# A fused attention and MLP kernel: chunks of 320 and 256 tokens, one chunk apart, and a layer norm by a matmul of ones

## What is computed

```python
scores = where(0 <= i - j < 128, q @ k.T / 8 - slope[h] * abs(i - j), -1e9)   # i, j: tokens
attn = softmax(scores)                      # exp(s - max) / (sum + 1e-9)
x = (attn @ v), heads side by side          # 576 x 512 for each batch
xn = (x - mean(x)) / sqrt(var(x) + 1e-6) * g_ln
y = x + relu(xn @ w_ch1) @ w_ch2            # 512 -> 2048 -> 512
h = relu(y @ w_in)                          # 512 -> 1024
c = conv_w[0]*h[t-1] + conv_w[1]*h[t] + conv_w[2]*h[t+1]
out = (h * sigmoid(c)) @ w_out              # 1024 -> 512
```

## Time and profile before

| | us |
|---|---|
| median of 3 runs | 835.26 (834.32 to 838.26) |
| span of the profiled execution | 834.8 |
| prologue, to the first MLP matmul | 89.0 |
| MLP of batch 0, with attention of batch 1 | 151.5 |
| MLP of batch 1, with attention of batch 2 | 140.3 |
| MLP of batch 2, with attention of batch 3 | 138.6 |
| MLP of batch 3 | 104.1 |
| second network | 211.4 |

### The profile page before, as it was taken

One profiled execution on the slowest core, in us unless ns is written; L12 is line 12 of the kernel. 1 busy time (PEld: TensorE's weight loads), 2 busy tenths in 40 slices (PEclk: granted clock), 3 DMA queues, 4 the chain that ended last, 5 costly groups with the idle time before them and its releaser, 6 DMA issues.

```text
span 834.8 us, 17035 instructions
## 1 busy us (share of the span) xinstructions
PE 786.3 (94%) x5792; PEld 765.4 (92%) x5792; DVE 547.0 (66%) x1510; ACT 385.0 (46%) x1063; POOL 171.7 (21%) x155
## 2 busy tenths in 40 slices
PE   4776788999999999999999999999999999999998
PEld 3665778999999999998999999999998999999998
DVE  4997677777367777645677754522229887788862
ACT  5775456565224655512556632122235444444442
POOL 4553675211011211101112200021120110111100
PEclk9676799999999999999999999999999999999999
DMA  5441554221122123013121201411312122221101
GB/s 154 106 130 48 156 162 127 60 78 43 58 65 66 38 71 101 8 58 102 29 71 51 86 8 61 134 58 54 89 49 76 31 79 78 78 78 47 59 22 44
DMA packets 64425, 60.81 MB, mean 73 GB/s; under 512 B 23904, under 2 KB 52576, under 8 KB 63840
## 3 DMA queue, kind: packets, MB, share of 16 engines
q1 hardware_dynamic: 64352, 59.87, 24.3%
HBM read 45.69 MB, written 14.16 MB: 72 GB/s over the span
## 4 chain that ended last, share of the span: by engine, by line
PE 69%; DVE 11%; issue 11%; POOL 3%; ACT 2%; DMA 2%; SPq 1%; POOLq 0%; DVEq 0%; ACTq 0%
PE bank L1009 20%; PE bank L1011 19%; PE bank L1010 19%; PE bank L950 4%; PE bank L964 3%; PE bank L980 3%; DVE prob L741 2%; DVE q_st L829 1%; DMA w_stage<-w 1%; DMA q_raw<-qT 1%; DVE ch_stage L741 1%; POOL rstd L482 1%; DVE rows L734 1%; ACT prob L562 1%; DVE rows L736 1%
## 5 line engine op out<-in xcount | busy, mean ns | idle before, releaser
L1009 PE MATMUL bank<-h_hi,wb_hi 128*128 128x288 f32 x512 | 156.9, 306 | 3.1 <-DVE h_lo L798 2.3
L1009 PE MATMUL bank<-xn_hi,wa_hi 128*128 128x288 f32 x512 | 157.0, 307 | 2.7 <-issue 1.4
L1010 PE MATMUL bank<-xn_lo,wa_hi 128*128 128x288 f32 x512 | 152.0, 297 | 0.0
L1011 PE MATMUL bank<-xn_hi,wa_lo 128*128 128x288 f32 x512 | 152.0, 297 | 0.0
L1011 PE MATMUL bank<-h_hi,wb_lo 128*128 128x288 f32 x512 | 151.6, 296 | 0.0
L1010 PE MATMUL bank<-h_lo,wb_hi 128*128 128x288 f32 x512 | 151.5, 296 | 0.0
L798 DVE SCALAR_TENSOR_TENSOR h_lo<-bank,h_hi 128x288 fp32r<-128x288 f32 x128 | 58.1, 454 | 109.8 <-ACT h_hi L594 108.5
L594 ACT ACTIVATE h_hi<-bank 128x288 fp32r<-128x288 f32 x128 | 52.3, 409 | 164.1 <-PE bank L1011 163.1
L1009 PEld LDWEIGHTS bank<-h_hi,wb_hi 128*128 128x128 f32 x512 | 97.1, 190 | 5.2 <-issue 3.9
L1009 PEld LDWEIGHTS bank<-xn_hi,wa_hi 128*128 128x128 f32 x512 | 97.6, 191 | 4.0 <-issue 3.2
L1010 PEld LDWEIGHTS bank<-xn_lo,wa_hi 128*128 128x128 f32 x512 | 97.7, 191 | 0.0
(11 more groups left out here) (95 smaller groups left out, 1752.0 us busy)
## 6 DMA issues: line engine op xcount, KB each, us to landing
k_raw<-kT SPq DMA_DIRECT2D x64, 144.0 KB, 2.8
q_raw<-qT SPq DMA_DIRECT2D x64, 144.0 KB, 2.9
w_stage<-w SPq DMA_DIRECT2D x32, 256.0 KB, 3.0
x_in<-x_spill SPq DMA_DIRECT2D x8, 580.0 KB, 4.3
ch_in<-ch_spill SPq DMA_DIRECT2D x8, 580.0 KB, 5.2
x_spill<-xT SPq DMA_DIRECT2D x4, 1152.0 KB, 5.3
ch_spill<-ch_stage SPq DMA_DIRECT2D x32, 144.0 KB, 1.9
out<-out_stage SPq DMA_DIRECT2D x32, 144.0 KB, 1.8
```

The costliest lines, as they stand in the source:

```text
L1009: nc.tensor.matmul(dst, w_h, a_h, start=start, stop=False)
L1010: nc.tensor.matmul(dst, w_h, a_l, start=False, stop=False)
L1011: last = nc.tensor.matmul(dst, w_l, a_h, start=False, stop=stop)
```

## The change

**Chunks.** The tokens of a batch are now cut at 320 (T = 320, 256), for attention as for the MLP. Chunk 0 has the queries 0 to 319 with the keys 0 to 319 (three tiles), chunk 1 the queries 320 to 575 with the keys 192 to 575 (two tiles). Attention runs one chunk ahead of the MLP, not one batch. The prologue holds attention of batch 0's chunk 0; `first` the MLP of that chunk with attention of chunk 1; a loop of three turns has the phases `one` (MLP on 256 tokens of batch b, attention on 320 of batch b + 1) and `zero` (MLP on 320, attention on 256); `last` is the last MLP of 256 tokens. Heads are 3.2 slots apart in a phase of 32 slots, and a head's transposes stand 2.4 slots, its outputs 3.8 slots behind its scores. Raw q and k, v_st and prob have two buffers each; pt_hi, pt_lo and o_lo one.

**Layer norm.** GpSimd and VectorE sum xT over its four blocks of channels (x_sum); a float32 matmul with a matrix of 1/512 gives the mean in every partition; VectorE subtracts it (xc), and xc itself is split into xc_hi and xc_lo and goes into the MLP. ScalarE squares xc, GpSimd sums, a second such matmul gives the variance. It goes through three small DMAs and a power on 64 partitions to a row of 1/std for all partitions (move_var, store_rstd, load_rstd), which multiplies the MLP's output (it may, as relu commutes with a positive factor): two blocks on VectorE out of PSUM, two on GpSimd after a copy by ScalarE. GpSimd then adds xT, and the sum is stored once (y_spill), so that the second network loads one input and sums nothing.

**Weights.** 8 tiles are prepared in the prologue, 24 in `first`.

```diff
-LT = 96
-NORM_TIMES = {("IN", 0): 0.0, ("IN", 1): 1.0, ("OUT", 0): 3.0, ("IN", 2): 3.51, ("OUT", 1): 4.5, ("OUT", 2): 5.5}
-FIRST_NORM, FIRST_HEAD, HEAD_SLOTS, LAST_NORM = 0.0, 6.5, 5.2, 55.5
-LAG = {"S": 0, "PT": 1, "O": 1}
-W_PROLOGUE = 10
+T = (320, 256)
+TILES = ([(128, 0, 128, 128, 0), (128, 0, 256, 0, 128), (64, 128, 192, 0, 384)],
+         [(128, 0, 256, 0, 0), (128, 128, 256, 0, 256)])
+HEAD0, HEAD_SLOT = 0.8, 3.2
+AT = {("S", 0): 0.0, ("S", 1): 0.3, ("PT", 0): 2.4, ("O", 0): 3.8}
+VAR_AT, MEAN_AT = 6.0, 28.0
+AT_PROLOGUE = {("S", 0): 0.0, ("S", 1): 0.02, ("PT", 0): 1.04, ("O", 0): 1.4}
+W_PROLOGUE = 8
...
+        def phases(run, eng):
+            run("prologue", None, 0)
+            run("first", 0, 0)
+            with eng.Fori(0, B - 1) as b:
+                run("one", b, b + 1)
+                run("zero", b + 1, b + 1)
+            run("last", B - 1, None)
...
+            def mean(kind, bm, b):
...
+                nc.tensor.matmul(dst[:, 0:T[c]], ones[:], x_sum[:, 0:T[c]], start=True, stop=True).then_inc(bank_filled, 1)
+            def variance(kind, bm, ba):
...
+                nc.tensor.matmul(dst[:, 0:T[c]], ones[:], xc[:, 0, 0:T[c]], start=True, stop=True).then_inc(bank_filled, 1)
...
+            def sum_squares(b, c):
+                g = chunk_no(b, c)
+                pool.wait_ge(square_ready, g + 1)
+                nc.gpsimd.tensor_tensor(xc[:, 0:2, 0:T[c]], xc[:, 0:2, 0:T[c]], xc[:, 2:4, 0:T[c]], ALU.add).then_inc(square_step, 1)
+                pool.wait_ge(square_step, 2 * g + 1)
+                nc.gpsimd.tensor_tensor(xc[:, 0, 0:T[c]], xc[:, 0, 0:T[c]], xc[:, 1, 0:T[c]], ALU.add).then_inc(square_step, 1)
...
+            def add_residual(b, c):
...
+                pool.wait_ge(ch_act, g + 1)
+                pool.wait_ge(rstd_loaded, 16 * (g + 1))
+                nc.gpsimd.tensor_tensor(y_stage[:, 2:4, 0:T[c]], y_stage[:, 2:4, 0:T[c]],
+                                        rstd[:, 0:T[c]].unsqueeze(1).broadcast_to((P, 2, T[c])), ALU.mult).then_inc(ch_scaled, 1)
...
+                nc.gpsimd.tensor_tensor(y_stage[:, :, 0:T[c]], y_stage[:, :, 0:T[c]], xT[:, :, t0:t1], ALU.add).then_inc(y_done, 1)
...
+            def centre(b, c):
...
+                for part in range(2):
+                    nc.vector.tensor_tensor(xc[:, 2 * part:2 * part + 2, 0:T[c]], xT[:, 2 * part:2 * part + 2, T0[c]:T0[c] + T[c]],
+                                            src[:, 0:T[c]].unsqueeze(1).broadcast_to((P, 2, T[c])), ALU.subtract).then_inc(xc_ready, 1)
...
+            def evacuate(b, c):
...
+                nc.vector.tensor_tensor(y_stage[:, 0:2, 0:T[c]], acc[:, 0:2, 0:T[c]],
+                                        rstd[:, 0:T[c]].unsqueeze(1).broadcast_to((P, 2, T[c])), ALU.mult).then_inc(ch_dve, 1)
```

More of the change, by code:

```diff
@@ L98, in norm_items @@
[L98 to L115, removed]
@@ L144, in mlp_groups @@
 def mlp_groups():
[L146 to L149, removed]
+    seq = [("A", 0), ("A", 1)]
+    for k in range(2, F1):
+        seq += [("B", k - 2), ("A", k)]
+    seq += [("B", F1 - 2), ("B", F1 - 1)]
     return [(g - 1 + half / 2, x + (half,)) for g, x in enumerate(seq) for half in (0, 1)]
+MLP_C = {"first": 0, "one": 1, "zero": 0, "last": 1}
+ATT_C = {"prologue": 0, "first": 1, "one": 0, "zero": 1}
 def timeline(kind):
@@ new lines, with use_base @@
+USES = {k: [x for _, x in timeline(k) if x[0] in ("S", "PT", "O", "MEAN", "VAR")]
+        for k in ("prologue", "first", "one", "zero", "last")}
+assert USES["first"] == USES["zero"]
+N_USES = {k: len(v) for k, v in USES.items()}
+PAIR = N_USES["one"] + N_USES["zero"]
+assert N_USES["first"] % 2 == 0 and N_USES["one"] % 2 == 0
+def use_base(kind, batch):
+    if kind == "prologue":
+        return 0
+    first = N_USES["prologue"]
+    if kind == "first":
+        return first
+    first += N_USES["first"]
+    if kind in ("one", "last"):
+        return first + PAIR * batch
+    return first + PAIR * (batch - 1) + N_USES["one"]
@@ L415, in _ @@
+            phases(run, sp)
             last = B - 1
@@ L520, in run @@
                         y_lo_part(a[0], a[0])
-            run("prologue", 0)
-            run("first", 0)
-            with pool.Fori(0, B - 2) as b:
-                run("steady", b + 1)
-            run("last", B - 1)
+                    if kind == "first" and name == "v_lo" and a[0] == 0:
+                        sum_squares(0, 0)
+            phases(run, pool)
+            add_residual(B - 1, 1)
             with pool.Fori(0, B - 1) as b:
@@ new lines, in prob_t_hi, with phase_of @@
+            def prob_t_hi(b, c, h):
+                hd = head_no(b, c, h)
+                if (n := before(b, c, h, "O")) is not None:
+                    act.wait_ge(bank_filled, n)
+                act.wait_ge(bank_filled, last_use(b, c, ("PT", h, 0)))
+                src = bank[bank_no(phase_of(b, c), ("PT", h, 0))]
+                nc.scalar.activation(pt_hi[:], src[:], ACT.Copy).then_inc(pt_hi_ready, 1)
+            def phase_of(b, c):
+                if isinstance(b, int) and b == 0:
+                    return "first" if c else "prologue"
+                return "zero" if c else "one"
```

1072 lines of the change are left out of this document (539 added, 533 removed).

## The result

The changed kernel takes 919.85 us (median of 4 runs, 916.87 to 922.79) against 835.43 of the kernel before beside it: a ratio of 1.101 with the interval 1.097 to 1.104, slower by 10%. The profiled execution has a span of 914.7 us, 79.9 more than before. The direction was forecast and the size was not: 854 was the number, 875 the end of the range.

A forecast was written before the change was run, and what follows sets the result against it. TensorE was taken as busy throughout the last MLP and second network, the prologue as bound otherwise. 834.8 - 11 + 13 - 17.5 + 6.6 + 22.5 + 6 + 0 + 1.4 + 1 - 3 = 853.8, so 854 us; range 827 to 875.

The forecast's parts named there:

- The cadence of 320 and 256 columns: MLP on TensorE: matmuls of 320 columns come 0.146 us apart, those of 256 columns 0.12.
- MLP matmuls at zero: MLP: 384 matmuls each of 320 and 256 columns cost the same as 768 of 288, change zero.
- The attention of batch 0's second chunk, +13: Chunk 1 of batch 0 leaves the prologue and enters TensorE's stream: 8 heads x 14 x about 0.116, +13.0 us.
- the old transposes: Layer norm: groups of 4 transposes leave TensorE's stream, 2.5 us a chunk for 7 chunks, -17.5 us.
- the new matmuls: Layer norm: 15 products with the matrix of ones enter TensorE's stream at 0.44 us each, +6.6 us (2 to 13).
- The prologue: Prologue on 320 tokens becomes one chain of 8.1 us a head; MLP starts at 78 us (73 to 83), -11.
- Phases `one` and `zero`: Loop: in-order chain makes heads 7.5 us apart in `one`, 7.4 in `zero`; +22.5 us (6 to 36) and +6 (0 to 15).
- rival C: GpSimd and VectorE exclude each other: first phase 9 us more, each phase `one` 3 us more; 872 us, chance 0.18.
- The 2 us of pt_hi behind GpSimd's residual: Start of phase `one`: residual delays v_lo(0) and v of head 1, so pt_hi(0) starts at 10.0 instead of 8.0 us.
- The first phase at no stall: First phase, with 24 weight tiles and twice the heads beside them: keeps 14 us of loss, change 0 (-5 to +9).
- The second network at 0: Second network loses VectorE's y_sum, covered by TensorE's full row: 0; differing from 211 us by over 1 means wrong.
- Rival A: Loop chains close in time, a head's period in phase `one` under 6.8 us, prologue period 7.6: 826 us, chance 0.2.

The follow-up runs named there:

- the normalisation ahead: Changed kernel with VectorE's normalisation 0.85 instead of 1.5 slots behind the scores beside the MLP, ahead of q_lo and xT: 864.07 us.
- the short k_lo: Changed kernel with GpSimd making only the first 8 columns of k_lo, the rest zero: 891.29 us; with the normalisation moved as well, 846.66 us.

## Why the prediction was wrong

The measured sum is 61 us above the forecast's. As the table counts, 17 us are stalls in the loop, 17 stalls in the first phase, 15 the MLP's own matmuls, 6 the prologue, 4 the layer norm, the rest small terms.

- **The cadence of 320 and 256 columns: right.** Undisturbed matmuls came 0.146 and 0.118 us apart; 0.146 and 0.12 were the forecast.
- **MLP matmuls at zero: wrong, +14.7.** I counted them undisturbed. A matmul ahead of a wait is followed only when it is over (0.28 us for 256 columns instead of 0.118), and by the profile that is no idle time: 53 such places against 12 before, +7 us. Stretches of matmuls at half their rate cost 10 us against 5 before. The first is the start of the first phase; in the others the granted clock was 0.50, six times in the phases of the changed kernel and three times with the normalisation ahead. Most of the rest, +4, are single matmuls behind transposes and outputs, followed after 0.2 us. In the stretch shown the granted clock was 0.50, the level of 1.2 GHz, with TensorE at 1.00 a few us earlier, and a wait of 1.85 us in between. That the waits brought these stretches is argued, not shown:

```profile
527.40:528.60 1.20, 1.20 (x13) 1.00 0.00 0
533.75:537.10 3.35, 3.35 (x18) 0.50 0.15 36
```

- **The attention of batch 0's second chunk, +13: right** (+12.4 in all, of which the first phase's attention is 11.9).
- **Layer norm: the old transposes right, the new matmuls too cheap by 2 us.** The forecast counted the delay up to the second next matmul. So counted, the 42 groups of transposes cost 17.6 us, and 17.5 were taken off; the 15 products with the matrix of ones cost 8.9 us, where I had 6.6. The timeline of TensorE in the last chunk, one such product (a line of two records) among the MLP's:

```profile
664.42 0.28 PE L1027 MATMUL bank<-xc_hi,wa_lo 128*128 128x256 f32 x1
664.54 0.59 PE L1021 MATMUL bank<-xc,ones 128*128 128x256 f32 x2
664.78 0.47 PE L1025 MATMUL bank<-xc_hi,wa_hi 128*128 128x256 f32 x1
665.09 0.28 PE L1026 MATMUL bank<-xc_lo,wa_hi 128*128 128x256 f32 x1
```

  From 664.54 to 665.09 are 0.55 us, of which 0.12 are the MLP matmul's own: 0.43 us for a product of 256 columns. The next start alone (0.24) hides almost half of it, since the matmul behind is followed after 0.31 us. A product of 320 columns costs 0.64 so counted. The Trainium skill (FP8 and Floating Point Precision, TensorE Precision Notes) has four passes for true FP32, which would be 0.47 and 0.59 at this cadence (an estimate); the trace agrees.
- **The prologue: right mechanism, period too short.** Scores 8.8 us apart against 8.1 make 4 of the 6 us, and the steps behind the last scores took 18.2 us against 16.5. GpSimd's instructions stretched the multiplications, k_lo's and the weight tiles': the short k_lo took 7.6 us off the prologue, two weight tiles fewer 2.7. It was 84.1 us against a range that ended at 83.
- **Phases `one` and `zero`: the step that failed is the chain's price.** I named the chain and its order, and gave it 5.05 us from the end of a head's first scores to its transposes; on average it took 5.9 in the phases `one`. q_lo was priced at 0.45 us and took 0.80: it stands beside k_lo, which starts 0.3 us ahead of it. The exponentials were priced at 1.33 and took 1.56, as in two of seven heads a relu of the MLP stands between them. The multiplications were right at 0.93 on average (0.97); in the head shown they took 1.18 beside v_lo. I had used the contention for rival C with 3 us a phase, and left it out of the forecast's own chain. The stalls are 9.9 to 11.2 us in front of the transposes of a phase `one`, not 5.5, and 4.9 in a `zero`, not 2. The 2 us of pt_hi behind GpSimd's residual did not show.
- **The first phase at no stall: wrong, 16.6 us.** I kept the loss of 14 us of the kernel before and took it for the weights' whole price, so the chain of the loop had no stall in this phase. The phase went from 91.4 to 84.9 us with the normalisation ahead, and to 76.0 with the weights' pace at 1.05 slots too: part is the same order, part the pace.
- **The second network at 0: +1.15, just beyond the 1 us that I had named as a sign of being wrong.** TensorE idles 3.5 us in it, 1.9 before, in waits for ScalarE; the cause was not looked for.
- **Rival A (the chains close) did not come true for the order given** (8.6 us a head in a phase `one`, not under 6.8), but a single number of the order brings 55.8 us of the 84. Rival C named the contention, which is a part of the cause (the short k_lo brought 28.6 us alone, 17.4 with the normalisation ahead), and its 872 has not half of the size.

## What to carry to other kernels

Price a chain of in-order rows with the contention in it, and give every stall twice: its idle time, and the drain, restart and slower clock around it (here 63.6 us of idle time brought some 15 more). When a consumer waits at nearly every turn, look which instruction of its producer's row has no need to stand first, before anything is called a lack of throughput; here one number gave 56 of 84 us. A later place for the consumer was the weaker cure here, 36 us, as it brought a wait for a bank.

When costs are read from a timeline, the next start is not always the whole: count up to the second next instruction, as the products with ones show.

## What the runs showed of the hardware

- The multiplications and q_lo, VectorE's work from SBUF to SBUF, stretch beside GpSimd's (three multiplications 0.77 us alone and 3.23 beside three GpSimd instructions, q_lo 0.49 and 0.91); h_lo, which reads PSUM, does not (0.42 and 0.49 us beside GpSimd as alone, on average 454 to 456 ns in four runs).
- A float32 matmul that is no transpose stands in the trace as two records, and delays the matmuls behind it by 0.43 us for 256 columns and 0.64 for 320, about four times their cadence.
- In the changed kernel's prologue the column of the granted clock says 1.00, while 256 columns are 0.21 us apart, as in the kernel before at half clock. The trace has no record of the clock before 89.9 us, so that there the column can't be read as the clock.
- A back edge of the hardware loop cost TensorE 1.8 to 2.1 us in the changed kernel (1.44 before), and a `zero` of the first two turns was 2.9 us shorter without the loop.
